# A fused attention and two-layer MLP kernel: VectorE's order in the first unit, a split of x in two parts, and k turned back in quarters of the array

## The reference

```python
for t in range(S):
    state = alpha[:, :, t, :, None] * state + np.einsum('bhd,bhe->bhde', k[:, :, t], v[:, :, t])
    y[:, :, t] = np.einsum('bhd,bhde->bhe', q[:, :, t], state)
x = y.transpose(0, 2, 1, 3).reshape(B * S, H * D)
h = x @ w_in                       # 384 -> 2048
x = (np.maximum(h, 0) ** 2) @ w_out    # 2048 -> 384
h = x @ w2_in
out = (h / (1 + np.exp(-h))) @ w2_out
```

## Time and profile before

| | us |
|---|---|
| median of 3 runs | 902.41 (902.32 to 903.88) |
| the profiled execution | 901.92 |
| its span | 900.2 |
| TensorE busy | 882.8 (98% of the span) |
| VectorE busy | 419.6 (47%) |
| ScalarE busy | 399.1 (44%) |
| GpSimd busy | 65.9 (7%) |

### The profile page before, as it was taken

How to read it: one execution, slowest core, us unless ns; L and a number is a source line. 1 busy time by engine, 2 the same in 40 slices (tenths; PEclk the granted TensorE clock), 3 DMA queues, 4 the chain that set the end, 5 groups by cost and what they waited for, 6 DMA issues and landing times.

```text
span 900.2 us, 16185 instructions
## 1 busy us (share of the span) xinstructions
PE 882.8 (98%) x6346; PEld 723.4 (80%) x6346; DVE 419.6 (47%) x907; ACT 399.1 (44%) x710; POOL 65.9 (7%) x97
## 2 busy tenths in 40 slices
PE   7989979999999999999999999999999999999998
PEld 6767767887887788788888888888888888888898
DVE  7588966677777667773334312212212212212310
ACT  4765554455445445544666623333333323233520
POOL 2454300000000000001133000000000000000000
PEclk9999979999999999999999999999999999999999
DMA  9995325324233432301332200200200101100100
GB/s 156 227 227 115 80 66 128 85 65 111 69 71 82 110 81 64 101 19 54 105 105 90 88 1 0 71 1 1 71 0 22 50 1 36 35 1 1 36 11 28
DMA packets 106228, 59.94 MB, mean 67 GB/s; under 512 B 56416, under 2 KB 99808, under 8 KB 106144
## 3 DMA queue, kind: packets, MB, share of 16 engines
q1 hardware_dynamic: 100784, 51.84, 24.0%
q0 software_dynamic: 2048, 6.29, 2.3%
q10 hardware_dynamic: 3312, 0.69, 0.6%
HBM read 45.02 MB, written 9.44 MB: 60 GB/s over the span
## 4 chain that ended last, share of the span: by engine, by line
PE 90%; DVE 1%; issue 0%; DMA 0%; SPq 0%; ACT 0%; DVEq 0%; ACTq 0%
PE h_ps L829 42%; PE z_ps L843 39%; PE y_ps L861 2%; PE y_ps L806 1%; PE y_ps L737 1%; PE y_ps L724 1%; PE job_ps L715 1%; PE y_ps L814 1%; PE z_ps L861 1%; PE job_ps L861 1%; PE y_ps L715 0%; DVE kp L1180 0%; DMA x_raw<-y_sb 0%; DVE decay L1221 0%; SPq L446 0%
## 5 line engine op out<-in xcount | busy, mean ns | idle before, releaser
L1324 DVE TENSOR_TENSOR g_lo<-g,g_hi 128x512 fp32r<-128x512 f32 x177 | 122.3, 691 | 342.8 <-ACT g_hi L1044 243.0
L829 PE MATMUL h_ps<-x_hi,win_hi 128*128 128x512 f32 x576 | 227.8, 395 | 4.6 <-DVE x_lo L1316 3.6
L829 PE MATMUL h_ps<-x_hi,win_lo 128*128 128x512 f32 x576 | 225.1, 391 | 0.0
L829 PE MATMUL h_ps<-x_lo,win_hi 128*128 128x512 f32 x576 | 224.9, 390 | 0.0
L1039 ACT ACTIVATE g<-h_ps 128x512 f32<-128x512 f32 x96 | 57.4, 598 | 232.1 <-PE h_ps L829 232.1
L1041 ACT ACTIVATE g<-h_ps 128x512 f32<-128x512 f32 x96 | 57.3, 597 | 177.8 <-PE h_ps L829 177.7
L829 PEld LDWEIGHTS h_ps<-x_hi,win_hi 128*128 128x128 f32 x576 | 108.5, 188 | 28.6 <-issue 4.0
L829 PEld LDWEIGHTS h_ps<-x_hi,win_lo 128*128 128x128 f32 x576 | 108.5, 188 | 23.0
L829 PEld LDWEIGHTS h_ps<-x_lo,win_hi 128*128 128x128 f32 x576 | 108.6, 189 | 21.8
L843 PE MATMUL z_ps<-g_hi,wout_hi 128*128 128x512 f32 x288 | 116.8, 406 | 0.0
L1044 ACT ACTIVATE g_hi<-g 128x512 fp32r<-128x512 f32 x177 | 111.9, 632 | 5.7
(11 more groups left out here) (180 smaller groups left out, 890.3 us busy)
## 6 DMA issues: line engine op xcount, KB each, us to landing
z_scratch<-z_sb SPq DMA_DIRECT2D x18, 256.0 KB, 2.6
x_raw<-z_scratch SPq DMA_DIRECT2D x6, 768.0 KB, 4.5
v_sb<-in_v SPq DMA_DIRECT2D x44, 96.0 KB, 2.6
out_x<-z_sb SPq DMA_DIRECT2D x80, 48.0 KB, 1.7
nat_a<-in_alpha SPq DMA_DIRECT2D x40, 88.0 KB, 2.3
nat_k<-in_k SPq DMA_DIRECT2D x40, 88.0 KB, 2.4
nat_q<-in_q SPq DMA_DIRECT2D x40, 88.0 KB, 2.3
nat_a<-in_alpha SPq DMA_DIRECT2D x40, 80.0 KB, 2.4
```

Source lines behind the costliest of these rows:

```text
L829: last = nc.tensor.matmul(h_ps[f % 2][:], w[:, f, tile(kk)], x[par][:, kk, :], start=(kk == TILES[0] and n == 0), stop=(kk == TILES[-1] an ...
L1324: nc.vector.tensor_tensor(low, g[f % 2][:], high.bitcast(F32), ALU.subtract).then_inc(g_lo_made, 1)
```

## The change

Four things are changed.

1. **VectorE's list in unit 0.** For pair 4 the state is brought forward ahead of pair 5's scans. For pairs 6, 7 and 8 `a_turn` moves between the first instruction of the state update (`decay_stage`) and the rest. Pair 7's y is added at the start of step 14, and pair 8's q is turned one step later than its k.
2. **x in two parts.** At f = 14 the row tiles 2 and 1 are split into x_hi and x_lo, at f = 15 row tile 0. This holds for all of units 0 to 4.
3. **Pair 8's S job** stands in step 16 between the products, its I job behind them.
4. **k turned back in quarters.** For pairs 4 and later, 16 matmuls with the identity, of 48 rows, 64 output partitions and 48 columns, write the turned k behind the scores into the same two banks. The masks wait for them, and the copy `kt_copy` waits for the masks.

```diff
@@ stage_step, behind
     if n == 2 * PAIRS:
-        return {"A": 13, "KQ": 14, "S": 15, "I": 16, "Y": 17}[kind]
+        return {"A": 13, "KQ": 14, "S": 16, "I": 16, "Y": 17}[kind]
...
-    return kind == "S" and n in (PAIRS, 2 * PAIRS) or kind == "I" and n not in (PAIRS, 2 * PAIRS)
+    return kind == "S" and n == PAIRS or kind == "I" and n > PAIRS
@@ TensorE, s_stage and s_halves
                 if n >= PAIRS:
                     s_halves(n)
-                    t_stage(n)
                     return
...
+                wait(pe, kt_copied, n)
+                for b in range(BATCH):
+                    for half in (0, 1):
+                        cols = slice(b * P + half * HALF, b * P + (half + 1) * HALF)
+                        for h in (0, 1):
+                            r, at = head_rows(h), BATCH * HALF + b * HD
+                            last = nc.tensor.matmul(job_ps[1 + h][half * HALF:(half + 1) * HALF, at:at + HD],
+                                                    kp[n % 2][r, cols], ident[r, r], start=True, stop=True,
+                                                    skip_group_check=True)
+                last.then_inc(kt_made, 1)
@@ ScalarE
             def kt_copy(n):
                 wait(act, i_made, n)
                 wait(act, kt_made, n + 1)
...
+                wait(act, masked, 2 * (n + 1))
+                at = BATCH * HALF
+                nc.scalar.activation(kp_t[:].rearrange("s b (h d) -> s h b d", h=2)[:, :, :, 0:HD],
+                                     s_ps[:].rearrange("s (h x) -> s h x", h=2)[:, :, at:at + BATCH * HD].rearrange(
+                                         "s h (b d) -> s h b d", b=BATCH), ACT.Copy).then_inc(kt_copied, 1)
...
+            def split_x_first(par, units):
+                wait(act, y_moved[0], moved(units + 1, 0))
+                wait(act, y_moved[1], moved(units, PAIRS - 1))
+                for kk in TILES[:-1]:
+                    split_x_tile(par, kk)
+            def split_x_last(par, units):
+                wait(act, y_moved[1], moved(units + 1, 1))
+                split_x_tile(par, TILES[-1])
...
                 if f == SPLIT_STEP and u + 1 < UNITS:
-                    split_x((u + 1) % 2, ys=u + 2)
+                    split_x_first((u + 1) % 2, u + 1)
+                if f == SPLIT_STEP + 1 and u + 1 < UNITS:
+                    split_x_last((u + 1) % 2, u + 1)
@@ VectorE, s_stage
                 if n >= PAIRS:
+                    wait(dve, kt_made, n + 1)
@@ VectorE, the loop over F
+                for kind, n in jobs_here:
+                    if kind == "Y" and n == 2 * PAIRS - 1:
+                        y_stage(n)
                 for kind, n in jobs_here:
                     if kind == "S":
                         s_stage(n)
                     if kind == "KQ":
                         k_stage(n)
-                        q_stage(n)
+                        if n != 2 * PAIRS:
+                            q_stage(n)
+                if F == stage_step("KQ", 2 * PAIRS) + 1:
+                    q_stage(2 * PAIRS)
+                if F == stage_step("I", PAIRS):
+                    decay_stage(PAIRS)
+                    i_stage(PAIRS)
+                    a_scan(PAIRS + 1)
+                    a_grow(PAIRS + 1)
                 low_g(u, f, g_pair(F), u >= UNITS, NF * u)
...
+                if F == stage_step("A", PAIRS + 1):
+                    a_turn(PAIRS + 1)
...
-                for kind, n in beside(F):
-                    if kind == "A" and n > PAIRS:
-                        a_stage(n)
+                for kind, n in jobs_here:
+                    if kind == "I" and n > PAIRS:
+                        decay_stage(n)
+                for kind, n in jobs_here:
+                    if kind == "A" and n > PAIRS + 1:
+                        a_turn(n)
+                for kind, n in jobs_here:
+                    if kind == "I" and n > PAIRS:
+                        i_stage(n)
+                for kind, n in jobs_here:
+                    if kind == "A" and n > PAIRS + 1:
+                        a_scan(n)
+                        a_grow(n)
...
-                if f == SPLIT_STEP and u + 1 < 2 * UNITS:
+                if f == SPLIT_STEP and u + 1 < UNITS:
+                    split_x(u + 1, (u + 1) % 2, TILES[:-1])
+                if f == SPLIT_STEP + 1 and u + 1 < UNITS:
+                    split_x(u + 1, (u + 1) % 2, TILES[-1:])
+                if f == SPLIT_STEP and UNITS <= u + 1 < 2 * UNITS:
                     split_x(u + 1, (u + 1) % 2)
```

More of the change, by code:

```diff
@@ L243, in build @@
         z_ps = [bank(f"z_ps{i}") for i in range(KD)]
-        y_ps = ctx.enter_context(nc.psum_tensor("y_ps", [P, 2 * 512], F32))
-        job_ps = [y_ps[:, 512:1024], bank("job_ps1")[:, :], y_ps[:, 0:512]]
+        jobs = ctx.enter_context(nc.psum_tensor("jobs", [P, 3 * 512], F32))
+        s_ps, y_ps = jobs[:, 0:1024], jobs[:, 512:1536]
+        job_ps = [jobs[:, 1024:1536], jobs[:, 0:512], jobs[:, 512:1024]]
         token_ps = [*job_ps, z_ps[0]]
@@ L718, in s_halves @@
                 last.then_inc(s_made, 1)
+                wait(pe, kt_copied, n)
[8 more added lines that the diff above has]
+                last.then_inc(kt_made, 1)
             def t_stage(n):
                 wait(pe, kt_copied, n)
-                wait(pe, i_copied, min(n, PAIRS))
+                wait(pe, i_copied, n)
                 for b in range(BATCH):
@@ L794, in y_halves @@
                 wait(pe, decayed, n - PAIRS + 1)
-                wait(pe, kt_copied, n + 1)
+                wait(pe, i_copied, PAIRS)
                 v_flat = v_tile(n).rearrange("t b h d -> t (b h d)")
@@ L985, in kt_copy @@
                 wait(act, kt_made, n + 1)
-                nc.scalar.activation(kp_t[:], job_ps[0][:].rearrange("s (b d) -> s b d", b=BATCH)[:, :, 0:ROWS],
-                                     ACT.Copy).then_inc(kt_copied, 1)
+                if n < PAIRS:
+                    nc.scalar.activation(kp_t[:, :, 0:ROWS], job_ps[0][:].rearrange("s (b d) -> s b d", b=BATCH)[:, :, 0:ROWS],
+                                         ACT.Copy).then_inc(kt_copied, 1)
+                    return
+                wait(act, masked, 2 * (n + 1))
[3 more added lines that the diff above has]
+                                         "s h (b d) -> s h b d", b=BATCH), ACT.Copy).then_inc(kt_copied, 1)
             def y_copy(n):
@@ L1270, in s_stage, with i_parts, decay_stage @@
                                                 causal[:].unsqueeze(1).to_broadcast([P, BATCH, P]), ALU.mult).then_inc(masked, 1)
-            def i_stage(n):
-                p, count = n % PAIRS, n - PAIRS
-                old = state[:, p, :, 0:HD]
+            def i_parts(n):
+                p = n % PAIRS
                 first, second = (x.rearrange("d (b e) -> d b e", b=BATCH) for x in half_state)
[L1278 to L1282, removed]
+                factors = [half_rest[n % 2][:, half::2, 0:1].to_broadcast([ROWS, BATCH, HD]) for half in (0, 1)]
+                sums = [x[0:ROWS, 0:BATCH * HD].rearrange("d (b e) -> d b e", b=BATCH) for x in half_i]
+                return n - PAIRS, state[:, p, :, 0:HD], first, second, factors, sums
+            def decay_stage(n):
+                count, old, first, _, factors, _ = i_parts(n)
                 wait(dve, y_made, n)
@@ L1289, in i_stage @@
                     wait(dve, state_made, count - PAIRS + 1)
-                nc.vector.tensor_tensor(first, old, whole(0), ALU.mult).then_inc(first_decayed, 1)
+                nc.vector.tensor_tensor(first, old, factors[0], ALU.mult).then_inc(first_decayed, 1)
+            def i_stage(n):
+                count, old, first, second, factors, sums = i_parts(n)
                 wait(dve, i_made, n + 1)
                 wait(dve, first_decayed, count + 1)
-                nc.vector.tensor_tensor(second, sums(0), first, ALU.add).then_inc(first_added, 1)
+                nc.vector.tensor_tensor(second, sums[0], first, ALU.add).then_inc(first_added, 1)
                 wait(dve, first_added, count + 1)
-                nc.vector.tensor_tensor(second, second, whole(1), ALU.mult).then_inc(decayed, 1)
+                nc.vector.tensor_tensor(second, second, factors[1], ALU.mult).then_inc(decayed, 1)
                 if has_state(n):
                     wait(dve, decayed, count + 1)
-                    nc.vector.tensor_tensor(old, sums(1), second, ALU.add).then_inc(state_made, 1)
+                    nc.vector.tensor_tensor(old, sums[1], second, ALU.add).then_inc(state_made, 1)
             def y_stage(n):
@@ L1376, in _ @@
                     a_grow(PAIRS)
-                for kind, n in beside(F):
-                    if kind == "I":
-                        i_stage(n)
-                    if kind == "Y":
+                if F == stage_step("A", PAIRS + 1):
[8 more added lines that the diff above has]
+                    if kind == "I" and n > PAIRS:
+                        i_stage(n)
```

(9 more changed lines are left out.)

7 lines of the change are left out of this document (2 added, 5 removed).

## The result

The changed kernel takes 927.76 us (median of 4 runs, 926.97 to 928.56), the kernel before beside it 902.92 (902.32 to 903.88): a ratio of 1.0274, with a 95% interval of 1.0256 to 1.0292. The profiled execution took 928.33 us, its span 926.7. TensorE is the bound as before, and is now idle at the ends of units.

What follows compares the result with a forecast made beforehand. TensorE, busy 882.8 of 900.2 us, was taken as the bound. Terms 1.8 + 2.6 + 23.2 + 0.1 = 27.7 us on 901.92 gave 929.6, or 930.1 at the median; own range 926 to 934, eight in ten 921 to 935.

Steps and rivals of the forecast that it cites:

- The ends of units 1 to 3: TensorE waits 5.09 us for the third x_lo, plus 2.65 for the clock: 7.74 us an end, 23.2 for three.
- the fall: Granted clock halves for a while with each stall at a unit's end, costing 2.65 us each.
- The end of unit 0: Step 17's first product ends at 131.25 against 128.65, 2.6 us later, pairs 4 to 8 included.
- VectorE's shift: In unit 0 by step 14, VectorE 0.35 us later; bounds 0.5 earlier and 0.9 later.
- The quarters: Turning k in quarters costs 0.12 us more a pair, 1.8 us for the fifteen pairs 9 to 23.
- The waits: TensorE waits for x_lo four times, about 22 us; score waits gone; one y_sb wait, about 2 us, at pair 5.
- rival 4: A second wait behind each stall, as S waits for late k and q: 2 us at four places, 938; chance 0.06.
- The clock: The windows behind each stall show a clock of 0.5 for some 5 us.
- Rival 1: Stalls at the ends of units without any fall of the clock: 922.2 us; chance 0.13.
- Rival 2: Faster: the third x_lo is in time at the ends of units, 896.7 us; chance 0.03.
- Rival 3: Quarters are dear: their matmuls don't overlap, 0.47 us more in 20 pairs, 939.5 us; chance 0.04.
- covered: In units 1 to 4, masks waiting 0.46 us more for the turned k, and the copy behind them, delay nothing.

Runs made afterwards that it cites:

- experiment 1: The changed kernel with the third x_lo ahead of the A job instead of behind it: 901.14 us, ratio 0.9983 to the kernel before.
- experiment 5: The changed kernel with the third x_lo between the A job's scans back and scans forward: 918.72 us, ratio 1.0163 to the kernel before.
- experiment 4: The changed kernel with 64 unneeded matmuls filling TensorE's wait for the last x_lo at the ends of units 0, 1 and 2: 919.58 us, ratio 1.0199.
- experiment 3: The kernel before with only the turning of k in quarters added, masks waiting for it: 905.09 us, ratio 1.0036 to the kernel before.
- experiment 2: The changed kernel with k turned back by the old full-size transposes, masks no longer waiting for it: 926.07 us, ratio 1.024 to the kernel before.
- experiment 8: experiment 1's kernel with pair 9's A job moved in unit 0 behind pair 8's masks and state: 903.23 us, ratio 1.0007 to the kernel before.
- experiment 9: experiment 7's kernel with only pair 9's scans forward moved behind pair 8's masks and state: 897.00 us, ratio 0.9937 to the kernel before.
- experiment 7: The changed kernel with the third x_lo ahead of the A job and the old full-size transposes: 897.60 us, ratio 0.9942 to the kernel before.
- experiment 6: The kernel before with only VectorE's new list in unit 0 and pair 8's S job moved: 901.38 us, ratio 0.998 to the kernel before.
- experiment 10: experiment 9's kernel with unit 0's third x_lo also ahead of step 15's g_lo: 897.13 us, ratio 0.9937 to the kernel before.

## Why the prediction was right, step by step

**The number.** 930.1 was forecast, 927.76 measured. 27.7 us were to be added; the last product ends 24.65 us later, 25.21 counted from pair 4's S job. The mechanism came as forecast (the A job ahead of the third x_lo, four stalls, a fall of the clock with each). Most terms were put somewhat too high.

**The ends of units 1 to 3**, forecast 7.74 us each. From the end of the product ahead to the end of the next first product the distance grew by 7.99 us at unit 1 (from 1.67 late to 9.66 late: 200.98 against 199.31, and 218.44 against 208.78). At units 2 and 3 it grew by 7.2 and 6.6. The stall itself was forecast 5.09; the seventh matmul would have started at 202.55 + 1.67 = 204.22 and started at 209.17, 4.95. Experiment 1 shows that it is the A job ahead of x_lo, experiment 5 that it shrinks with what is taken away, experiment 4 that the remainder is the clock. The term of the sum that was mis-sized is the fall: I took 2.65 for each, from one fall seen before, and it was 2.9, 2.1 and 1.5, 6.5 us instead of 8.0.

The reason that I gave for adding a fall holds a misreading. I compared the stall of 5.09 us with 2.4 us of idle time before the fall in the kernel before. But TensorE had been idle for only 1.6 us there, took up pair 8's S job, and was busy all through 114.00 to 114.50, where the clock fell. That a fall came at every end is right, but those rows did not show that 2.4 us of idle time bring one.

**The end of unit 0**, forecast 2.6 us, measured 1.26 (129.91 against 128.65), or 1.8 counted from pair 4's S job. The list from pair 8's last scan to the third x_lo was as long as worked out: 12.2 us (107.18 to 119.33), against 12.3. But it began 1.7 us earlier than put. The step that failed is VectorE's shift: I had it 0.35 us late at step 14. Pair 8's scans started at 103.38, against 104.70 before. Of these 1.3 us, 0.56 are the earlier start of this execution, which is chance; the other 0.8 go with the new order. Pair 7's masks came no later than before (99.04 against 99.21), or 0.4 us later counted from pair 4's S job, and what was lost there was more than won back by the turned a, which fills VectorE's wait for I (101.41, ahead of 102.34). On the other side, the fall of the clock cost 3.3 us here, 0.7 more than put: two errors of this term partly cancel.

**The quarters**, forecast 0.12 us a pair, 1.8 in all: 0.10 a pair and 1.6 in all by the chain behind unit 0 (experiment 3), with line 726 at 0.45 us and the product behind it at 2.27. The Trainium skill says in "TensorEngine Tiling (Array Packing)", under "Key Properties", that changing the tiling mode drains the engine. The trace agrees: the full-size product takes 2.27 us behind quarters and 2.04 behind full-size work, so nothing is gained when quarters replace full-size transposes just ahead of a product.

**The waits.** Forecast were four waits for x_lo, 22 us, three of 5.1 and one of about 7; the view has 21.1 in four, the longest 6.6, the others 4.8. The wait of about 2 us for y_sb at pair 5 is there (1.8), the score wait is gone, and no second wait stands behind the stalls (rival 4). **The clock**: half rate at each stall as forecast, but for 10.2, 6.8, 6.8 and 3.4 us at the ends of units 0 to 3 rather than for about 5 each time. **Rival 1** (no fall, 922.2) fails by these windows, and experiment 4 shows what it would have been worth. **Rival 2** (faster, 896.7) needed the A job elsewhere; experiment 1 puts it there and gets 901.1, and with the transposes undone too, 897.6. **Rival 3** (dear quarters) fails by experiments 2 and 3.

One thing was left out of the working: that after a stall is removed, the masks behind pair 9's A job, and ScalarE's new wait for them, become the next wait in unit 0 (2.0 us in experiment 1). I had called it covered, and looked at units 1 to 4 alone, where that holds.

## What to carry to other kernels

When an operand is split into parts to let its first parts go early, look at where the last part lands in its engine's list: the consumer needs all of it at nearly the same moment, and one long job ahead of the last part undoes the whole. A wait of the engine that bounds the kernel costs its own length, and then often a stretch at half clock, here 1.5 to 3.3 us on top of 4.8 to 6.6; price the two apart. When two profiles are compared, look first at a moment ahead of every change: here it lay up to 2 us apart, as much as the quarters cost in all. Where moving a job frees one wait, look for what is queued behind the job in its new place, as experiments 8 and 9 show.

## What the runs showed of the hardware

The granted clock can fall after the idle time is over: in experiment 5 TensorE went on at 206.86 and the clock came down in the window from 207.50, with TensorE busy. In the kernel before it fell with TensorE at work too. A shorter gap (2.69 us rather than 4.80) did not spare it. A gap of 1.8 to 2.0 us, the wait for y_sb at pair 5, did both: in the profiles of experiments 2, 5, 7 and 9 half rate of 3.4 us followed it, and in those of the changed kernel and of experiments 1, 4, 6, 8 and 10 none. Equal stalls of 4.8 us went with half rate of different length: 3.4 us at the end of unit 3, nearly 7 at the ends of units 1 and 2. What a fall costs goes by the time at half rate in which TensorE has work, and is a little under half of it. From the end of the stall it was about 7.5, 6.5, 4.7 and 3.4 us at the ends of units 0 to 3, and the costs were 3.3, 2.9, 2.1 and 1.5; at unit 2 the clock had been down for 2 us of the stall already. The Trainium skill ("TensorE: Matmul & The Clock Gate", the caveats under "Seeing it yourself") warns that recorded clock events may be unreliable. Here they agree with the durations: where the windows have 0.50, the second product took 3.65 to 4.13 us, and 2.27 to 2.29 where they have 1.00, and filling the idle time removed both together.

Matmuls that nothing needs paid for themselves: 64 of them made the kernel 7 to 8 us faster than the same kernel without them. It is a repair, not a cure, since removing the stalls was worth nearly 27 (experiment 1).
